# Attention stage: gate values made chunk by chunk inside the loop, state rows scaled on ScalarE, output gates by tanh

## Reference, cut to what matters

```
B, H, S, D = 4, 8, 768, 40
for t in range(S):
    m_new  = max(f_gate[t] + m, i_gate[t])
    f_stab = exp(f_gate[t] + m - m_new);  i_stab = exp(i_gate[t] - m_new);  m = m_new
    C = f_stab * C + i_stab * outer(v[t], k[t])
    n = f_stab * n + i_stab * k[t]
    y[t] = sigmoid(o_gate[t]) * (C @ q[t]) / max(|n . q[t]|, 1)
x = y as [3072 tokens, 320];  x = moe(x);  out = moe2(x)
```

## Time and profile before

| what | value |
|---|---|
| median of 3 runs | 804.44 us (802.71 to 804.91) |
| the profiled execution | 811.87 us, of which 810.2 us are its span |
| mean granted TensorE clock | 0.957 |
| attention stage | from the start to about 208 us |
| first `rden` (unit 0) to last (unit 47) | 34.69 to 203.63 us |
| busy over the span | PE 707.8, DVE 549.8, POOL 341.0, ACT 294.2 us |

### The profile page before, as it was taken

The page is one execution under the profiler, slowest core; times in us unless marked ns, Lnnn a source line. Parts: engine busy times, 40 slices in busy tenths (PEclk is TensorE's granted clock), DMA queues, the critical chain, the costliest instruction groups (busy, mean ns, idle before and its releaser), DMA issues. The chain is left out here.

```text
span 810.2 us, 16421 instructions
## 1 busy us (share of the span) xinstructions
PE 707.8 (87%) x4855; PEld 627.9 (78%) x4855; DVE 549.8 (68%) x1666; ACT 294.2 (36%) x743; POOL 341.0 (42%) x484
## 2 busy tenths in 40 slices
PE   0799999999435799888899999987999999999996
PEld 0699999999324695776777887873989899899996
DVE  5569899998677777777888756464536366455652
ACT  4322222222013442241635446451524255344440
POOL 7568887787003322140615326342324134240441
PEclk9999999999557999999999999999999999999998
DMA  8956667761642423231343352344653335451610
GB/s 274 176 155 187 190 184 188 194 187 38 206 124 65 158 80 95 79 119 62 79 136 120 103 173 88 134 145 159 221 157 117 119 108 165 148 164 57 201 35 19
DMA packets 99639, 109.56 MB, mean 135 GB/s; under 512 B 39053, under 2 KB 83726, under 8 KB 99568
## 3 DMA queue, kind: packets, MB, share of 16 engines
q1 hardware_dynamic: 88384, 84.27, 36.2%
q0 software_dynamic: 4080, 12.61, 4.8%
q10 hardware_dynamic: 7104, 11.80, 4.4%
HBM read 89.45 MB, written 20.02 MB: 135 GB/s over the span
## 5 line engine op out<-in xcount | busy, mean ns | idle before, releaser
L566 POOL TENSOR_TENSOR parts_w2l<-all_w,parts_w2h 128x320 fp32r<-128x320 f32 x128 | 111.8, 898 | 275.6 <-ACT parts_w2h L553 275.2
L640 DVE SCALAR_TENSOR_TENSOR l_hl<-bank,l_hh 128x384 fp32r<-128x384 f32 (+1 forms) x138 | 78.0, 566 | 93.4 <-ACT l_hh L636 92.0
L636 ACT ACTIVATE l_hh<-bank 128x384 fp32r<-128x384 f32 (+1 forms) x138 | 69.0, 500 | 132.6 <-PE bank L607 127.9
L603 PE MATMUL bank<-l_xh,parts_w1h 128*128 128x384 f32 x256 | 89.5, 350 | 11.2 <-DVE l_hl L640 9.8
L604 PE MATMUL bank<-l_xl,parts_w1h 128*128 128x384 f32 x256 | 86.3, 337 | 0.0
L605 PE MATMUL bank<-l_xh,parts_w1l 128*128 128x384 f32 x256 | 86.3, 337 | 0.0
L560 DVE TENSOR_TENSOR parts_w1l<-all_w,parts_w1h 128x384 fp32r<-128x384 f32 x128 | 77.6, 638 | 1.1 <-ACT parts_w1h L546 0.7
L627 PE MATMUL bank<-parts_w2h,l_hh 128*128 128x320 f32 x232 | 75.1, 324 | 0.7 <-DVE l_hl L640 0.5
L628 PE MATMUL bank<-parts_w2l,l_hh 128*128 128x320 f32 x232 | 72.3, 312 | 0.0
L629 PE MATMUL bank<-parts_w2h,l_hl 128*128 128x320 f32 x232 | 72.3, 312 | 0.0
L1434 PE MATMUL bank<-parts_w2h,l_hh 128*128 128x320 f32 x192 | 67.5, 351 | 3.5 <-issue 1.9
(11 more groups left out here) (269 smaller groups left out, 1728.9 us busy)
## 6 DMA issues: line engine op xcount, KB each, us to landing
all_w<-in_moe_w SPq DMA_DIRECT2D x16, 1024.0 KB, 5.4
all_w<-in_moe_w SPq DMA_DIRECT2D x10, 1280.0 KB
all_w<-in_moe_w SPq DMA_DIRECT2D x32, 256.0 KB, 6.4
all_w<-in_moe_w ACTq DMA_DIRECT2D x6, 1280.0 KB
att_kT<-in_kT SPq DMA_DIRECT2D x24, 256.0 KB, 2.8
att_qD<-in_qT SPq DMA_DIRECT2D x48, 128.0 KB, 3.1
att_qT<-in_qT SPq DMA_DIRECT2D x24, 256.0 KB, 3.2
rows<-parts_pad SPq DMA_DIRECT2D x8, 483.0 KB, 7.1
```

The source lines that it names most:

```text
L566: ops.tensor_tensor(sh.w2l[:, r, p, :], sh.w2[:, p, :], sh.w2h[:, r, p, :].bitcast(FP), ALU.subtract).then_inc(sh.w2_low, 1)
L603: T.matmul(dst, sh.w1h[:, r, k, f], xh[:, k, :], start=k == 0, stop=False)
L636: return nc.scalar.activation(hh, src, ACT.Relu)
L640: return nc.vector.scalar_tensor_tensor(hl, src, 0.0, hh.bitcast(FP), ALU.max, ALU.subtract)
```

## The change

- **Gates per chunk.** Only chunk 0 is made ahead of the loop, on 96 x 128 elements. The values of chunk c+1 are made inside chunk c: DVE scans in units 0 and 2, POOL does one subtraction or addition in units 0, 1, 2 and 4 and two in unit 3, ACT makes the bf16 parts in units 2, 4 and 5 and copies the transposed values out in unit 4, PE transposes in unit 4.
- **Output gates.** SP loads them one batch entry at a time, ACT applies tanh(x/2) and then 0.5x + 0.5 in even units, in place of the sigmoid ahead of the loop.
- **Scaling of the state rows** (`inter`) moves from one DVE instruction to four on ACT, one for each head, each with a scale per partition taken from eG. `keep_logits` moves from DVE to ACT too. DVE's `readout` waits for `inter_done` before it updates C.
- **Start.** PE runs 9 dense products of ones before the first transposes, and 2 and 4 more in the two steps ahead of the loop. Half of the zeroing of qD moves to ACT, that of C and xs to DVE.
- **Routing constants** move into the last chunk (POOL unit 1, DVE and ACT unit 2).

```diff
-            sp.dma_start(gate[:, :, :].rearrange("p g t -> p (g t)"), a["gates"]).then_inc(in_gate, 16)
+            gates = a["gates"].rearrange("p (g t) -> p g t", t=S)
+            sp.dma_start(gate[:, :, 0:P], gates[:, :, 0:P]).then_inc(in_first, 16)
             tile_load(0, 0, True)
+            sp.dma_start(gate[:, :, P:2 * P], gates[:, :, P:2 * P]).then_inc(in_second, 16)
+            tile_load(0, 1, True)
+            gate_load(0, 0)
             sp.dma_start(wg[:, :, :, :].rearrange("p g j e -> p (g j e)"), a["w_gates"]).then_inc(in_wg, 16)
-            for b in range(1, B):
+            for b in range(2, B):
                 tile_load(0, b, True)
+                gate_load(0, b - 1)
+            gate_load(0, B - 1)
+            sp.dma_start(gate[:, :, 2 * P:], gates[:, :, 2 * P:]).then_inc(in_gate, 16)
             with sp.Fori(1, NC) as c:
                 for b in range(B):
                     tile_load(c, b, False)
+
+                    sp.wait_ge(gate_o, c * B - B + b + 1)
+                    gate_load(c, b)
...
+            def decay_steps(n):
+
+                before = m[:, bass.ds(n * P - 1, P)]
+                pool.wait_ge(m_done, n + 1)
+                pool.wait_ge(G_done, n)
+                pool.sem_inc(pool_carry, 1)
+                nc.gpsimd.tensor_tensor(lf[:, :], fg[:, chunk(n)], before, ALU.add).then_inc(sum_done, 1)
+
+            def decay_differences(n):
+
+                pool.wait_ge(sum_done, n + 1)
+                pool.sem_inc(pool_carry, 1)
+                nc.gpsimd.tensor_tensor(lf[:, :], lf[:, :], m[:, chunk(n)], ALU.subtract).then_inc(lf_done, 1)
+
+            def column_half(n):
+
+                pool.wait_ge(m_done, n + 1)
+                pool.sem_inc(pool_carry, 1)
+                nc.gpsimd.tensor_tensor(col[:, :], ig[:, chunk(n)], m[:, chunk(n)], ALU.subtract).then_inc(col_half, 1)
+
+            def columns(n):
+
+                pool.wait_ge(G_done, n + 1)
+                pool.wait_ge(col_half, n + 1)
+                nc.gpsimd.tensor_tensor(col[:, :], col[:, :], G[:, :], ALU.subtract).then_inc(col_done, 1)
+
+            def part_rest(n, i):
+
+                pool.wait_ge(part_done, 3 * n + i + 1)
                 if i:
-                    pool.wait_ge(rest_done, i)
-                    pool.wait_ge(parts_done, i)
-                nc.gpsimd.tensor_copy(G_parts[band, :], (G, *rest)[i][band, :]).then_inc(parts_done, 1)
-            pool.wait_ge(parts_done, 3)
-            pool.wait_ge(colT_done, 1)
+                    pool.wait_ge(rest_done, 2 * n + 1)
+                pool.sem_inc(pool_carry, 1)
+                rows = upto[i + 1]
+                left = rest[0][rows, :] if i else G[rows, :]
+                nc.gpsimd.tensor_tensor(rest[i][rows, :], left, G_parts[rows, chunk(n)], ALU.subtract).then_inc(rest_done, 1)
...
+                pool.wait_ge(gate_o, c * B + b + 1)
...
+                if k == 0 and not last:
+                    decay_steps(c + 1)
+                if k == 1 and not last:
+                    decay_differences(c + 1)
+                if k == 2 and not last:
+                    pool.wait_ge(gates_T, c + 1)
+                    column_half(c + 1)
+                if k == 3 and not last:
+                    columns(c + 1)
+                if k in (3, 4) and not last:
+                    part_rest(c + 1, k - 3)
+                if k == 1 and last:
+                    routing_constants(nc, sh)
                 if k >= 0:
                     finished(c, k)
 
+            column_half(0)
+            columns(0)
...
+            def decayed_rows(c, k):
+
+                u = c * UPC + k
+                h0, par = k * HU, k % 2
+                if k == 0:
+                    act.wait_ge(eG_done, c + 1)
+                wait_done(act, O_psum, u)
+                wait_done(act, num_done, u - 1)
+                act.sem_inc(act_carry, 1)
+                for h in range(HU):
+                    x = nc.scalar.activation(inter[:, h, :], p_O[par][:, (HU + h) * V1:(HU + h + 1) * V1], ACT.Copy,
+                                             scale=eG[:, bass.ds(c * BH + (h0 + h), 1)])
+                x.then_inc(inter_done, 1)
+
...
+            def gate_part(n, i):
+
+                if i:
+                    act.wait_ge(rest_done, 2 * n + i)
+                else:
+                    act.wait_ge(G_done, n + 1)
+                act.sem_inc(act_carry, 1)
+                left = rest[i - 1][upto[i], :] if i else G[:, :]
+                nc.scalar.activation(G_parts[upto[i], chunk(n)], left, ACT.Copy).then_inc(part_done, 1)
+
+            def output_gates(c, b):
+
+                i = c * B + b
+                act.wait_ge(in_o[b], c * 16 + 16)
+                act.sem_inc(act_carry, 1)
+                x = X[:, bass.ds(i + 1, 1), :].rearrange("p i n -> p (i n)")
+                nc.scalar.activation(x, x, ACT.Tanh, scale=0.5).then_inc(gate_half, 1)
+                act.wait_ge(gate_half, i + 1)
+                act.sem_inc(act_carry, 1)
+                nc.scalar.activation(x, x, ACT.Copy, bias=0.5, scale=0.5).then_inc(gate_o, 1)
+
             def step(c, k, last):
                 if not (last and k + 2 >= UPC):
                     weights(c, k + 2)
-                if k >= 0 and k % 2 == 0:
+                if k < 0:
+                    return
+                if k in (4, 5) and not last:
+                    gate_part(c + 1, k - 3)
+                decayed_rows(c, k)
+                if k == 4 and not last:
+                    gate_columns(c + 1)
+                if k % 2 == 0:
+                    output_gates(c, k // 2)
                     copy_xT(c, k)
-
...
+                else:
+                    keep_logits(c, k - 1)
+                if k == 2 and not last:
+                    gate_part(c + 1, 0)
+                if k == 2 and last:
+                    routing_ends(nc, act, sh)
...
-                op = p_O[par][:, 0:2 * HU * V1].rearrange("p (w h e) -> p w h e", w=2, e=V1)
-                e = eG[:, bass.ds(c * BH + k * HU, HU)].unsqueeze(2).to_broadcast([P, HU, V1])
-                wait_done(dve, y_done, u - QB)
-                nc.vector.tensor_tensor(inter[:, :, :], op[:, 1, :, :], e, ALU.mult).then_inc(inter_done, 1)
+                wait_done(dve, inter_done, u)
                 wait_done(dve, Cd_done, u)
                 for j, half in enumerate(halves):
                     x = nc.vector.tensor_tensor(C[half, k, :, j * V1:(j + 1) * V1], Cd[half, k % QB, j::2, :],
                                                 p_O[par][half, 2 * HU * V1:(2 * HU + PR) * V1].rearrange("p (r e) -> p r e", e=V1),
                                                 ALU.add)
                 x.then_inc(C_done, 1)
-                wait_done(dve, inter_done, u)
-                nc.vector.tensor_tensor(num[:, k % QB, :, :], op[:, 0, :, :], inter[:, :, :], ALU.add).then_inc(num_done, 1)
+                wait_done(dve, y_done, u - QB)
+                op = p_O[par][:, 0:HU * V1].rearrange("p (h e) -> p h e", e=V1)
+                nc.vector.tensor_tensor(num[:, k % QB, :, :], op, inter[:, :, :], ALU.add).then_inc(num_done, 1)
...
+                if k == 2 and last:
+                    routing_codes(nc, dve, sh)
+                if k == 0 and not last:
+                    decay_max(c + 1)
+                if k == 2 and not last:
+                    dve.wait_ge(gates_T, c + 1)
+                    dve.wait_ge(rest_done, 2 * c + 2)
+                    decay_sums(c + 1)
...
+            def busy(n):
+                for _ in range(n):
+                    nc.tensor.matmul(p_O[1][:, :], sh.ones_b[:, :], sh.ones_b[:, :].unsqueeze(1).to_broadcast([P, HU, P]),
+                                     start=True, stop=True)
+
+            def gate_transposes(n):
+
+                pe.wait_ge(col_done, n + 1)
+                pe.sem_inc(pe_carry, 1)
+                nc.tensor.transpose(p_T[:, 0:BH], col[0:BH, :], ident[0:BH, 0:BH])
+                nc.tensor.transpose(p_T[:, BH:2 * BH], G[0:BH, :], ident[0:BH, 0:BH]).then_inc(gates_T, 1)
...
+                if k == 4 and not last:
+                    pe.wait_ge(eG_done, c + 1)
+                    gate_transposes(c + 1)
+                if k < 0:
+                    busy(6 + 2 * k)
...
+            busy(9)
+            pe.wait_ge(dg, 3)
+            gate_transposes(0)
+            pe.wait_ge(zeroed, 1)
+            pe.wait_ge(half_zeroed, 1)
             steps(pe, step)
```

More of the change, by code:

```diff
@@ L105, in routing_codes, with routing_ends @@
     V.scalar_tensor_tensor(sh.code_p[:, :], sh.code_p[:, :], 0.0, sh.code_p[:, :], ALU.is_equal, ALU.add)
+def routing_ends(nc, act, sh):
+    act.wait_ge(sh.lists_made, 6 + NE)
+    for g in range(2):
+        nc.scalar.activation(sh.prefix[:, g, NT:], sh.slot_col[:, 0:1].to_broadcast([P, 2]), ACT.Copy, scale=0.5)
 def attention(nc, a, sh):
@@ L293, in _ @@
             for x in act_sems:
[L294 removed]
+                act.sem_inc(x, LEAD - (x is xT_done or x is L_done))
```

(19 more changed lines are left out.)

155 lines of the change are left out of this document (68 added, 87 removed).

## The result

| | median | runs | granted clock |
|---|---|---|---|
| before | 803.58 us | 801.44 to 804.91 | 0.957 (profiled execution) |
| changed | 825.09 us | 818.24 to 831.74 | 0.918 to 0.938 |

The ratio is 1.0242 [1.0171, 1.0313]: the changed kernel is slower by 2.4%, and the time lies 7 us above the predicted range. The profiled execution of the changed kernel is its slowest (831.74, span 830.0); the ratio is made from the other three.

A forecast was written before the change was run, and what follows sets the result against it. TensorE bound the kernel before at 3.47 us a unit; a new 3.72 us ring would bind it after. Loop loss 17.1 less start gain 17.9 gives -0.8 us: 804 us, no change, range 785 to 818.

The forecast's parts named there:

- The start: Ahead of the loop: unit 0's reciprocal starts at 16.5 to 16.9 us against 34.69, a gain of 17.9.
- The ring: Each loop unit: log weights, exponentials, four scalings and readout follow one another, 3.72 us against TensorE's 3.47.
- The gate chain: Gate steps inside five chunks: delays on VectorE and ScalarE cost 1.6 us a chunk, 8.0 in all, bounds 2 and 16.
- chunk ends: After each chunk's branch: VectorE's idle 0.45 us, hidden behind TensorE before, now counts; 2.3 us in all.
- the last units: Units 46 and 47: 5.56 us becomes 6.3, with scalings in place of VectorE's multiplication in the last.
- Nor does TensorE gain or lose: it waits in the difference.: In each loop unit: TensorE idles between its 3.47 us and the 3.72 us unit, at no cost; two extra transposes fit.
- low-clock rival: At the start: TensorE is at 1.2 GHz, unit 0 costs 1.4 us more, three units take 6.4; 813 us, chance 0.15.
- It lies 7.4 above the median, which I carry over.: Whole kernel: the profiled execution's 7.4 us excess is kept constant, so 804.44 - 0.8 gives 804 us.
- The ring doesn't bind: Loop rival: scalings take 0.5 us, so TensorE stays the bound at 3.47 a unit; about 785 us, chance 0.15.
- GpSimd holds VectorE in every unit: Loop rival: small VectorE instructions wait for GpSimd, 0.25 us in 45 units, + 11; 815 us, chance 0.15.
- TensorE starts at 1.2 GHz: The low-clock rival by its claim: low level at the start, + 9.4 us, 813 us, chance 0.15.

The follow-up runs named there:

- experiment 3: The changed kernel with TensorE filler products of ones: five ahead of each pair of gate transposes in the loop, two behind the outputs of every other unit; 810.07 us.
- Experiment 10: The changed kernel with inter multiplied on VectorE again and TensorE's gate transposes behind the outputs of unit 4 instead of ahead; 791.75 us.
- Experiment 4: The kernel before with only VectorE's inter multiplication replaced by four scalings on ScalarE, no gate transposes in the loop; 835.98 us.
- experiment 13: The kernel before with three extra additions of 128x164 out of PSUM per unit on VectorE, into tiles nobody reads; 828.47 us.
- experiment 14: The changed kernel with two products of ones behind the outputs of every unit but a chunk's fifth, none ahead of the gate transposes; 810.85, 846.14, 857.62 and 873.15 us.
- experiment 9: The kernel before, unchanged, run again for a second profile; 803.88 us.
- experiment 1: The changed kernel with inter multiplied on VectorE again in one instruction, so ScalarE has no scalings; 800.18 us.
- experiment 2: The changed kernel with five products of ones ahead of each pair of gate transposes in the loop, nowhere else; 825.66 us.

## Why the prediction was wrong, by its own steps

**The start: 0.6 us late, within its bounds.** L534 of unit 0 at 17.48, predicted 16.5 to 16.9, and L614 at 0.35. Of the 0.6 above it, 0.3 is L530, which GpSimd's first addition held already in unit 0 (0.48 us at 16.77).

**The ring: right.** L499 to L360 0.72, to L363 0.07, to the first scaling 0.52, four scalings 0.85 (predicted 0.90; one takes 0.30), to the readout 0.09, to the next L499 1.45. Sum 3.70, predicted 3.72. In the Trainium skill's figures ("ScalarE: Activation LUTs", section "What ACT_TABLE_LOAD costs") the four would take an estimated 0.97; the trace is 0.12 below that.

**The gate chain, chunk ends and the last units: right in sum.** 31.98 us for a chunk against 31.8, and 184.7 against 186.0 for the loop, once the clock is held (experiment 3).

**The step that failed: "Nor does TensorE gain or lose: it waits in the difference."** I costed TensorE's idle time at nothing. It has a price, because the granted clock doesn't always stay up through it. Experiment 3 took most of the idle time away with added work and the kernel got 15.0 us faster (825.1 to 810.1). Experiment 10 took it away without any filler and has no fall either. Experiment 4 brings a fall into the kernel before by the scalings alone, and experiment 13 brings falls by VectorE alone. The four runs of the changed kernel agree: by span x (1 - clock) / 0.5 they hold 136, 124, 112 and 101 us at the low level for 831.7, 826.4, 823.8 and 818.2 us, about 0.39 us lost for each; those of experiment 3 hold 69 to 80. My low-clock rival looked at the start only ("It decides at one unit at the low level"), where it did not happen. The Trainium skill's rule that I cited beside it ("TensorE: Matmul & The Clock Gate", section "What's actually happening"), that the low level is the default and activity releases it, bore on the loop as much as on the start; I read it for one place. That the clock fell in the changed kernel's loop and not in experiments 3 and 10 agrees with it; the 89 us of experiment 14, in which TensorE was busy throughout at 0.50, don't.

**The second failure: the base.** "It lies 7.4 above the median, which I carry over." The 7.4 us were three units at the low level at the start of the loop, where the changed kernel is at the high level, and the ordinary execution doesn't have them (experiment 9). Against that one the start gains 33.03 - 17.5 = 15.5 and the loop loses 186.0 - 162.0 = 24.0, so the same working gives + 8.5: 812 us, slower, where I had said no change. Experiment 3, the changed kernel with its clock held, measures 810.1.

Together: 825.1 - 804.0 = 21.1. Of these 15.0 are the falls. The other 6.1 are the base, worth 8.4 by the working (812.4 - 804), less 2.3 for the rest, such as a loop of 184.7 instead of 186.0 and what follows the loop; with two medians in it, this division is good to a few us.

**The rivals.** "The ring doesn't bind" is out: VectorE waits 0.96 in each undisturbed unit; without the scalings, in experiment 1, the readout at 84.92 follows L507 with no wait. "GpSimd holds VectorE in every unit" is out: L530 takes 0.17 at 117.42, and 0.4 to 0.5 only in units with a gate step. "TensorE starts at 1.2 GHz" is out for the changed kernel.

**Left open.** Which gap brings a fall: waits of 0.5 to 1.5 us stood right ahead of falls, and others as long, up to 1.85 us in experiment 4, passed; runs of one kernel differ. Nor does the amount of idle time sort them: experiment 4's TensorE, busy for 0.86 of the 69 us before its fall, fell once, the changed kernel's, busy for 0.89 to 0.91, four times. Nor was it shown why a low stretch ends after 3.5 us here and after 89 there.

## What to carry to other kernels

Where TensorE is the bound, its spare capacity isn't free. A ring 7% longer than TensorE's unit, 11 us by my sum, cost 31.4 in experiment 4: some 20.8 in longer units and chunk ends, and some 10.6 because TensorE's granted clock fell in a gap and TensorE then set the pace again at half its clock. So a unit that grows from 3.47 to 3.7 us should be costed at the low level for part of the time, or the gaps closed: by moving a wait behind work that is ready (the gate transposes behind the outputs), or by filler: in every gap it held the clock here, at one gap alone or everywhere but there it didn't. And before the excess of a profiled execution over its median is carried over, look where in it the excess lies; if the change alters that place, it is no constant.

## What the hardware showed that I had not expected

- The granted clock fell to half behind idle times of 0.5 to 1.5 us in a stage where TensorE was otherwise busy, in nine of the kernels, and stayed low for 3.5 to 89 us, the 89 with TensorE busy throughout.
- The same wait of 1.20 us ahead of `x_transposes` that stood before a fall in experiment 2 passed without one at 23.1 us of the changed kernel.
- The clock column can miss a low stretch: for 28 to 46 us of the kernel before it says 1.00, while L480 takes 1.77 us and L485 0.50, as at the low level of the changed kernel, and not 0.98 and 0.35.
- At the low level the whole unit grows, not only TensorE's part: 6.0 to 6.8 us a unit, against 3.7 to 4.2, since VectorE and ScalarE then wait for it.
- An instruction on VectorE that reads PSUM ran in 0.33 us beside GpSimd's work, where the next one, between SBUF tiles, had taken 0.39 without it and then took 0.16.
